# FFT filter and routed experts: ranks, splits and a gather moved in the first expert blocks

## The chip, the cores and the metric

One core of a Trainium2 chip runs the whole program. The metric is the device time of one execution in microseconds (us); lower is better. The kernel before takes 497.0 us in the median of three runs (496.35 to 500.02).

## The reference

```python
X = np.fft.rfft(x, axis=1)                      # x: 8 x 3072 x 256
y = np.fft.irfft(X * (filt_r + 1j*filt_i), n=3072, axis=1)
x = y.reshape(24576, 256)
logits = x @ w_gate                             # 8 experts
idx = argmax(logits); gate_w = softmax(logits)[idx]
# every expert takes the first 768 tokens that chose it (in token order); others give 0
h = relu(disp @ w1)                             # per expert 768x256 @ 256x1024
y = h @ w2                                      # 1024x256
out[i] = gate_w[i] * y[expert of i, slot of i]
```

## The kernel before, in words

The rows of a batch are filtered in stages: a transform of length 128, a transform of length 24 with the product by the filter (`wide`, banks 4 and 5 of PSUM), the inverse, and back to rows. Since each expert takes only 768 tokens, the kernel does three batches (`FIRST = 3`), the third (`t == HALF`, 2) by half, and asks at the end whether all experts are full; the code under `r > 0` is for the case that they are not, and isn't run here.

Behind the batches come 16 expert blocks of 384 tokens (`BLOCKS`, `TOK`), two for each of the 8 experts. `spot(b)` gives expert and half: blocks 0 to 3 are experts 0, 1, 0, 1, then 4 and 5 are expert 2, 6 and 7 expert 3 and so on. Blocks 0 and 1 use only tokens of the first two batches; block 2 is the first that needs the routing of the third. What a block does:

- `pool_gather` (L1143, POOL): three indirect DMAs of 128 rows into `g_in[b % 2]`. It waits until the turn of two blocks before has freed the buffer.
- turn, `pe_block_turn` (L642, TensorE): six transposes into banks 0 and 1; ACT copies them to `xh` (L763), VectorE writes the remainder `xl` (L825).
- up(b) (L1255, TensorE): 8 tiles of 6 matmuls of 384 columns, round four banks (4, 5, 6, 7). The product in fp32 is made of three products of parts (`xh`, `xl` with `w1h`, `w1l`). ACT makes `hh` (L1034) of every tile, VectorE `hl` (L1083). Tile n waits for the `hl` of tile n-4. The turn of block b+1 stands before tile 6 in blocks 0 and 2, and behind up(b) in most others.
- down(b, s) (L1269, TensorE): 24 matmuls for each of three parts s, into banks 2 and 3 in turn; ACT scales by the gates to `o_out` (L1043, `downed`), and POOL stores the rows with an indirect DMA (L1171, `pool_sent`). The gates are fetched by `pool_gates` (L1155).

The weights of an expert are loaded raw by SP (`raw_load`, L981 for w1, L983 for w2; 1 MB each, one raw buffer for w1 and one for w2 from expert 1 on). ACT makes the high part (`act_split`, L995 for w1, L997 for w2), then `low_split` (L1005) the low part: VectorE for w1, POOL for w2 (from expert 1 on). The load for the next expert waits for the low split of the one before, since it overwrites its raw buffer: w1 of expert 3 is loaded only behind the low split of w1 of expert 2. Slot e % 2 of `w1h`, `w1l`, `w2h`, `w2l` holds expert e, so a w1 split of expert 2 may not start before up(2) is done (`h_done`), and a w2 split of expert 2 not before down(2) is done (`o_done`).

Order of the first blocks on TensorE (`pe_last`, `pe_experts`): products 0 to 3 of the third batch (L576, rows of y), turn(0), products 4 and 5, a wait until all y copies are out of banks 0 to 3, the rank matmuls (`pe_rank`, L591 and L592, into bank 3), up(0) with turn(1), up(1), down(0) parts 0 and 1, `pe_table` (L603, makes the token table of the third batch), down(0) part 2, down(1) parts 0 and 1, turn(2), down(1) part 2, up(2) with turn(3), up(3), turn(4), down(2), up(4), turn(5), down(3), and from there up(b), turn(b+1), down(b-1).

VectorE works off the routing of the third batch in `dve_route` steps between the `hl` of blocks 0 and 1 (`FIRST_ROUTE`, `NEXT_ROUTE`): steps 8 and 9 (L873, L877) behind the first `hl`, 10 and 11 behind the second, 12 (L886) and 13 behind the third, up to 21 (L907); the one-hot steps `hot_lo` (L912, three of them), L915, L918, L921 in block 1. `pe_table` waits for the last of them, and the tokens (L946) for gather 2 wait for `pe_table`.

Engine queues are in order. Each order is written by hand, so a wait holds back all that stands behind it in the same queue. POOL's order ahead of block 2: gathers 0 and 1, wait for tile 5 of up(0), gates 0, low split of w2 of expert 1, the store of the third batch's gates, gates 1, stores of block 0, gather 2, gather 3, stores of block 1, wait for tile 6 of up(2), gates 2, wait for tile 2 of up(3), gather 4, wait for tile 7, gates 3.

Of the kernel before, what the change touches and what calls it, by code (L numbers as in the profile page):

```python
# [29 lines left out]
HALF = FIRST - 1  # L30
# [164 lines left out]
def build(nc, x, fab_d, wg, w1, w2, wa_d, wf_d, wbi_d, wai_d, sq_d, tri_d, row_d, num_d, out):  # L195
# [4 lines left out]
    with ExitStack() as ctx:  # L200
# [80 lines left out]
        ps = [psum[:, i].rearrange("p k d -> p (k d)") for i in (0, 1, 4, 5, 2, 3, 6, 7)]  # L281
        work = [psum[:, i].rearrange("p k d -> p (k d)") for i in range(WORK + 1)]
        back = [psum[:, i].rearrange("p k d -> p (k d)")[:, 0:DH * 4 * HR] for i in (3, 6)]
# [160 lines left out]

        held = [None] * (WORK + 1)
        place_of = {"pe": 0, "act": 0}
# [198 lines left out]
        def place_of_row(t, i, engine):  # L645

            return 2 + (i - 4) if t == HALF and i >= 4 else next_work(engine)

        def pe_last(pe, t, r):
            pe_logits(pe, t, 0)  # L650
            pe_logits(pe, t, 1)
            for k, i in enumerate(half_order() if t == HALF else range(N2 // 2)):
                pe_turn_v(pe, t, i)
                if k == 1:
                    pe_raw(pe, t)
                if k == 3:
                    pe_route_in(pe, t)
            for i in range(products(t)):
                if r == 0 and i == 4:
                    for k in range(DH):  # L660
                        free_work(pe, k)
                    pe_block_turn(pe, r, 0)
                pe_product(pe, t, i, place_of_row(t, i, "pe"))
            for k in range(WORK + 1):
                free_work(pe, k)
            if r == 0:
                pe_rank(pe, t, 5)

# [351 lines left out]
        def act_experts(act, r, last):  # L1020
            def turned(b):
                act_block_turned(act, r, b)
# [23 lines left out]
            if r > 0:  # L1046
                turned(0)
            for b in range(BLOCKS):
                q, i = divmod(b, 4)
# [7 lines left out]
                if 0 < b < BLOCKS - 1 and b != 2:  # L1057
                    turned(b + 1)
                if b == 0:
                    act_split(act, r, 1, 1)  # L1060
                if i == 3 and more:
                    act_split(act, r, 2 * q + 3, 0)
                if i == 2 and more:
                    act_split(act, r, 2 * q + 2, 0)
# [4 lines left out]
                if i == 0 and q > 0:  # L1069
                    act_split(act, r, 2 * q + 1, 1)  # L1070
                if i == 3 and more:
                    act_split(act, r, 2 * q + 2, 1)
            downed(BLOCKS - 1)

        def dve_experts(dve, r, last):
# [34 lines left out]
            for b in range(2 if r == 0 else 0, BLOCKS):  # L1110
# [4 lines left out]
                if 0 < b < BLOCKS - 1 and b != 2:  # L1115
                    turned(b + 1)
                if i == 3 and more:
                    low_split(dve, r, 2 * q + 3, 0)
                if i == 2 and more:
                    low_split(dve, r, 2 * q + 2, 0)  # L1120
# [59 lines left out]
        def pool_last(pool, t, r):  # L1180
            gate_store(pool, t - 1)
            if r == 0:
# [5 lines left out]
                pool_gather(pool, r, 1)  # L1188
                pool_after(pool, r, 0, 5)
                pool_gates(pool, r, 0)  # L1190
                low_split(pool, r, 1, 1)
                gate_store(pool, t)
# [11 lines left out]
        def pool_experts(pool, r, last):  # L1204
# [10 lines left out]
            pool_sent(pool, r, 1)  # L1215
            pool_after(pool, r, 2, 6)
            pool_gates(pool, r, 2)
            pool_after(pool, r, 3, 2)
            pool_gather(pool, r, 4)
            pool_after(pool, r, 3, 7)  # L1220
            pool_gates(pool, r, 3)
# [15 lines left out]
        def pe_experts(pe, r, last):  # L1237
# [3 lines left out]
            def up(b):  # L1241
# [4 lines left out]
                for f in range(FT):  # L1246
                    if n * FT + f >= 4:
                        pe.wait_ge(hl_done, n * FT + f - 3)
                    if b in (0, 2) and f == TURN_AFTER:
                        turn(b + 1)  # L1250
# [31 lines left out]
            up(0)  # L1282
            up(1)
            down(0, 0)
            down(0, 1)
# [197 lines left out]
```

## Time and profile before

| what | us |
|---|---|
| median of 3 runs (lowest, highest) | 497.0 (496.35, 500.02) |
| the profiled execution: time | 496.46 |
| the profiled execution: span in the profile | 494.6 |
| TensorE busy | 453.8 (92% of the span) |
| VectorE, ACT, POOL busy | 243.0, 215.4, 188.8 |

The span runs from the first to the last instruction of the profile. Times inside it are counted from its start. "Busy" is the sum of the durations; an engine that is idle while another sets the end costs nothing. The mean granted clock of TensorE is 0.993 of full speed. The chain that ended last is the work followed backwards from the last instruction, at each step to what released it.

### The profile page before, as it was taken

Reading aid. Unit: us, or ns where it says so; the run is one execution under the profiler, and the core shown is the slowest. Engines: PE = TensorE matmul, PEld = TensorE weight load, DVE = VectorE, ACT = ScalarE, POOL = GpSimd, SP = SyncE. Lnnn points to the kernel's source line nnn. Section 1 sums busy time; section 2 is a strip of 40 time slices with the busy share of each in tenths; the row PEclk is TensorE's granted clock in tenths of the full one; section 3 lists DMA queues with packets and bytes.
Section 4 is the critical chain, followed back from the end, with each engine's and each line's share of the span. In section 5 each row is a group of like instructions: output and inputs, shape, how many; then the busy total and the mean of one; then the engine's idle time right before and its main releaser. Section 6 shows DMA issues by size and latency. Waiting matters only on the chain.

```text
span 494.6 us, 12093 instructions
## 1 busy us (share of the span) xinstructions
PE 453.8 (92%) x5160; PEld 399.2 (81%) x5160; DVE 243.0 (49%) x380; ACT 215.4 (44%) x402; POOL 188.8 (38%) x159
## 2 busy tenths in 40 slices
PE   5989999896998878989979999999999999999993
PEld 5855558555774464979969999999999999999993
DVE  1095526899499965791453242363134344224300
ACT  2745555351455546621544253455434345423310
POOL 0000000000000050386467887566786457584122
PEclk9999999998999999999999999999999999999998
DMA  8994989859943354822132794411795310970011
GB/s 301 404 401 137 345 260 323 290 205 329 320 136 120 136 209 129 279 87 86 43 118 66 239 404 167 138 45 33 242 403 184 129 43 27 345 268 23 33 35 36
DMA packets 45743, 93.02 MB, mean 188 GB/s; under 512 B 5840, under 2 KB 20848, under 8 KB 45168
## 3 DMA queue, kind: packets, MB, share of 16 engines
q1 hardware_dynamic: 39408, 79.50, 45.8%
q0 software_dynamic: 6272, 12.65, 7.7%
q8 instruction: 43, 0.70, 0.6%
q14 instruction: 20, 0.16, 0.1%
HBM read 46.49 MB, written 45.64 MB: 186 GB/s over the span
## 4 chain that ended last, share of the span: by engine, by line
PE 79%; DVE 12%; issue 4%; DMA 2%; ACT 1%; POOLq 0%; POOL 0%; SPq 0%; DVEq 0%; ACTq 0%
PE psum L1269 27%; PE psum L1255 25%; DVE prod L787 5%; PE psum L489 4%; PE psum L506 4%; PE psum L473 4%; PE psum L546 3%; PE psum L503 3%; PE psum L642 2%; PE psum L580 2%; PE psum L536 2%; PE psum L522 1%; DVE hot_lo L912 1%; DVE prod L795 1%; PE psum L576 1%
## 5 line engine op out<-in xcount | busy, mean ns | idle before, releaser
L1083 DVE SCALAR_TENSOR_TENSOR hl<-psum,hh 128x384 fp32r<-128x384 f32 x128 | 69.6, 556 | 144.4 <-ACT hh L1034 144.4
L1269 PE MATMUL psum<-w2h,hh 128*128 128x256 f32 x384 | 109.9, 286 | 0.0
L1269 PE MATMUL psum<-w2h,hl 128*128 128x256 f32 x384 | 108.8, 283 | 0.0
L1269 PE MATMUL psum<-w2l,hh 128*128 128x256 f32 x384 | 108.8, 283 | 0.0
L1034 ACT ACTIVATE hh<-psum 128x384 fp32r<-128x384 f32 x128 | 62.1, 492 | 61.5 <-PE psum L1255 61.3
L1255 PE MATMUL psum<-xh,w1h 128*128 128x384 f32 x256 | 86.2, 337 | 2.1 <-DVE hl L1083 2.0
L1255 PE MATMUL psum<-xh,w1l 128*128 128x384 f32 x256 | 85.7, 335 | 0.0
L1255 PE MATMUL psum<-xl,w1h 128*128 128x384 f32 x256 | 85.7, 335 | 0.0
L787 DVE TENSOR_TENSOR prod<-psum,fab 128x1024 f32<-128x1024 f32 x48 | 56.5, 1218 | 47.2 <-PE psum L473 38.9
L1171 POOL DMA_INDIRECT out<-o_out,token x48 | 50.2, 1047 | 70.5 <-ACT o_out L1043 56.7
L1269 PEld LDWEIGHTS psum<-w2l,hh 128*128 128x128 f32 x384 | 73.7, 192 | 0.0
L1269 PEld LDWEIGHTS psum<-w2h,hh 128*128 128x128 f32 x384 | 73.6, 192 | 0.0
L1269 PEld LDWEIGHTS psum<-w2h,hl 128*128 128x128 f32 x384 | 73.6, 192 | 0.0
L1143 POOL DMA_INDIRECT g_in<-y_rows,token x48 | 53.5, 1115 | 46.6 <-DVE token L946 32.3
L1043 ACT ACTIVATE o_out<-psum,o_gate 128x256 f32<-128x256 f32 x48 | 22.8, 475 | 108.3 <-PE psum L1269 108.3
L1155 POOL DMA_INDIRECT o_gate<-gate_rows,token x48 | 50.1, 1044 | 35.4 <-PE psum L1255 21.8
L1134 POOL DMA_DIRECT2D gate_rows<-gate x2 | 1.3, 660 | 145.3 <-DVE carry L883 145.3
L1255 PEld LDWEIGHTS psum<-xh,w1h 128*128 128x128 f32 x256 | 48.1, 188 | 3.0 <-DVE hl L1083 2.6
L1255 PEld LDWEIGHTS psum<-xl,w1h 128*128 128x128 f32 x256 | 48.1, 188 | 0.0
L1255 PEld LDWEIGHTS psum<-xh,w1l 128*128 128x128 f32 x256 | 48.1, 188 | 0.0
L489 PEld LDWEIGHTS psum<-wbi,prod 64*64 64x64 f32 x1536 | 34.4, 136 | 16.7 <-issue 9.8
L489 PE MATMUL psum<-wbi,prod 64*64 64x96 f32 x1536 | 39.5, 251 | 7.2 <-issue 3.3
(109 smaller groups left out, 540.7 us busy)
## 6 DMA issues: line engine op xcount, KB each, us to landing
out<-zero SPq DMA_DIRECT2D x24, 1024.0 KB, 12.3
w_raw<-in_w SPq DMA_DIRECT2D x14, 1024.0 KB, 5.8
x_in<-in_x SPq DMA_DIRECT2D x18, 512.0 KB, 6.4
t_scratch<-t_out SPq DMA_DIRECT2D x24, 256.0 KB, 4.1
z_in<-t_scratch SPq DMA_DIRECT2D x32, 192.0 KB, 3.9
y_rows<-y SPq DMA_DIRECT2D x12, 512.0 KB, 2.8
fab<-in_fab SPq DMA_DIRECT2D x4, 1024.0 KB, 14.4
first_raw<-in_w SPq DMA_DIRECT2D x2, 1024.0 KB, 8.2
```

Source lines behind the costliest of these rows:

```text
L473: mm = nc.tensor.matmul(wide[q * QR:(q + 1) * QR, a, c, :], wf[part(a), NQ * h + q, c, :], z_in[part(a), n % ZB, q, :], start=True, stop=True)
L489: mm = nc.tensor.matmul(back[q][part(low), at:at + 2 * HR], prod[part(q), n % 2, 0, a, c, d:d + A1], wbi[part(q), j, a, c, :], start=(c == ...
L506: mm = nc.tensor.matmul(work[k][:, :], wa[:, :], x_in[:, c, 2 * h:2 * h + 2, :], start=True, stop=True)
L787: nc.vector.tensor_tensor(prod[:, n % 2, f], wide, fab[:, h, :, f, :].unsqueeze(2).to_broadcast([P, 2, 2, D]), ALU.mult).then_inc(p_done, 1)
L1034: nc.scalar.activation(hh[:, b % 2, f, :], ps[(2, 3, 6, 7)[f % 4]][:, 0:TOK], ACT.Relu).then_inc(hh_done, 1)
L1043: nc.scalar.activation(o_out[:, b % 2, s, :], ps[4 + (b * ST + s) % 2][:, 0:D], ACT.Copy, scale=o_gate[:, b % 4, s:s + 1]).then_inc(o_evac, 1)
L1083: nc.vector.scalar_tensor_tensor(out=hl[:, b % 2, f, :], in0=ps[(2, 3, 6, 7)[f % 4]][:, 0:TOK], scalar=0.0, in1=hh[:, b % 2, f, :].bitcast ...
L1143: nc.gpsimd.indirect_dma_start(out=g_in[:, b % 2, s, :], out_offset=None, in_=yd[0:have], in_offset=bass.IndirectOffsetOnAxis(ap=tokens_of ...
L1155: nc.gpsimd.indirect_dma_start(out=o_gate[:, b % 4, s:s + 1], out_offset=None, in_=gd[0:have], in_offset=bass.IndirectOffsetOnAxis(ap=toke ...
L1171: nc.gpsimd.indirect_dma_start(out=out, out_offset=bass.IndirectOffsetOnAxis(ap=tokens_of(r, b, s), axis=0), in_=o_out[:, b % 2, s, :], in ...
L1255: mm = nc.tensor.matmul(ps[(2, 3, 6, 7)[f % 4]][:, 0:TOK], wt[k][:, h, f * P:(f + 1) * P], xx[:, b % 2, h, :], start=(m == 0), stop=(m == 5))
L1269: mm = nc.tensor.matmul(ps[4 + (b * ST + s) % 2][:, 0:D], hx[:, b % 2, f, s * P:(s + 1) * P], wt[k][:, f, :], start=(f == 0 and m == 0), s ...
```

## The change

- Banks: products 4 and 5 of the third batch go to banks 4 and 5 in place of 2 and 3. The rank matmuls go right behind turn(0), ahead of products 4 and 5, still in bank 3, which no product uses any more. The wait for all y copies ahead of them is gone; up(0) waits before tile 0 for the copy out of bank 4 and before tile 1 for that out of bank 5, and down(0) waits for banks 2 to 5.
- The w2 split of expert 1 (ACT) goes from behind the `hh` of block 0 to ahead of them. The low split that follows it on POOL goes ahead of gates 0, and POOL's wait for tile 5 of up(0) is gone.
- Gather 4 goes from behind tile 2 of up(3) to right behind the stores of block 1, ahead of gates 2; the waits for tile 6 of up(2) and tile 7 of up(3) are gone, that for tile 2 of up(3) stands now ahead of gates 3.
- The w1 split of expert 2 (ACT, and the low split on VectorE) goes from behind up(2) to behind up(3) and its turn(4). The w1 split of expert 3 goes on ACT from ahead of the `o_out` of block 2 to behind them, ahead of the w2 split of expert 2; its low split on VectorE goes from behind the `hl` of block 3 to behind those of block 4 and the `xl` of turn(5).

```diff
--- before.py
+++ after.py
@@ -279,7 +279,7 @@
 
         psum = ctx.enter_context(nc.psum_tensor("psum", [P, 8, 2, D], F32))
         ps = [psum[:, i].rearrange("p k d -> p (k d)") for i in (0, 1, 4, 5, 2, 3, 6, 7)]
-        work = [psum[:, i].rearrange("p k d -> p (k d)") for i in range(WORK + 1)]
+        work = [psum[:, i].rearrange("p k d -> p (k d)") for i in range(6)]
         back = [psum[:, i].rearrange("p k d -> p (k d)")[:, 0:DH * 4 * HR] for i in (3, 6)]
         wide = psum[:, 4:6]
         raw_at = P
@@ -442,7 +442,7 @@
                 for n in range(NG - 1, FIRST_ZEROS):
                     zeros(sp, n)
 
-        held = [None] * (WORK + 1)
+        held = [None] * 6
         place_of = {"pe": 0, "act": 0}
 
         def next_work(engine):
@@ -644,7 +644,7 @@
 
         def place_of_row(t, i, engine):
 
-            return 2 + (i - 4) if t == HALF and i >= 4 else next_work(engine)
+            return i if t == HALF and i >= 4 else next_work(engine)
 
         def pe_last(pe, t, r):
             pe_logits(pe, t, 0)
@@ -660,11 +660,11 @@
                     for k in range(DH):
                         free_work(pe, k)
                     pe_block_turn(pe, r, 0)
+                    pe_rank(pe, t, 5)
                 pe_product(pe, t, i, place_of_row(t, i, "pe"))
-            for k in range(WORK + 1):
-                free_work(pe, k)
-            if r == 0:
-                pe_rank(pe, t, 5)
+            if r > 0:
+                for k in range(WORK):
+                    free_work(pe, k)
 
         def act_a(act, t, i, first):
             c, h = divmod(i, 2)
@@ -1045,6 +1045,7 @@
 
             if r > 0:
                 turned(0)
+            act_split(act, r, 1, 1)
             for b in range(BLOCKS):
                 q, i = divmod(b, 4)
                 more = q < E // 2 - 1
@@ -1056,11 +1057,9 @@
                     downed(1, range(2))
                 if 0 < b < BLOCKS - 1 and b != 2:
                     turned(b + 1)
-                if b == 0:
-                    act_split(act, r, 1, 1)
-                if i == 3 and more:
+                if i == 3 and q > 0 and more:
                     act_split(act, r, 2 * q + 3, 0)
-                if i == 2 and more:
+                if i == 2 and q > 0 and more or b == 3:
                     act_split(act, r, 2 * q + 2, 0)
                 if b == 1:
                     downed(1, range(2, ST))
@@ -1068,6 +1067,8 @@
                     downed(b - 1)
                 if i == 0 and q > 0:
                     act_split(act, r, 2 * q + 1, 1)
+                if b == 3:
+                    act_split(act, r, 3, 0)
                 if i == 3 and more:
                     act_split(act, r, 2 * q + 2, 1)
             downed(BLOCKS - 1)
@@ -1114,9 +1115,9 @@
                     upped(b, f)
                 if 0 < b < BLOCKS - 1 and b != 2:
                     turned(b + 1)
-                if i == 3 and more:
-                    low_split(dve, r, 2 * q + 3, 0)
-                if i == 2 and more:
+                if i == 3 and q > 0 and more or b == 4:
+                    low_split(dve, r, 3 if b == 4 else 2 * q + 3, 0)
+                if i == 2 and q > 0 and more or b == 3:
                     low_split(dve, r, 2 * q + 2, 0)
 
         def tokens_of(r, b, s):
@@ -1186,9 +1187,8 @@
                 rows_ready(pool, t)
                 pool_gather(pool, r, 0)
                 pool_gather(pool, r, 1)
-                pool_after(pool, r, 0, 5)
+                low_split(pool, r, 1, 1)
                 pool_gates(pool, r, 0)
-                low_split(pool, r, 1, 1)
                 gate_store(pool, t)
                 pool_gates(pool, r, 1)
             else:
@@ -1213,11 +1213,9 @@
             pool_sent(pool, r, 0, range(ST - 1, ST))
             pool_gather(pool, r, 3)
             pool_sent(pool, r, 1)
-            pool_after(pool, r, 2, 6)
+            pool_gather(pool, r, 4)
             pool_gates(pool, r, 2)
             pool_after(pool, r, 3, 2)
-            pool_gather(pool, r, 4)
-            pool_after(pool, r, 3, 7)
             pool_gates(pool, r, 3)
             for b in range(2, BLOCKS - 1):
                 q, i = divmod(b, 4)
@@ -1246,6 +1244,8 @@
                 for f in range(FT):
                     if n * FT + f >= 4:
                         pe.wait_ge(hl_done, n * FT + f - 3)
+                    elif n == 0 and f < 2:
+                        free_work(pe, 4 + f)
                     if b in (0, 2) and f == TURN_AFTER:
                         turn(b + 1)
                     if b == 2 and f == 3:
@@ -1281,6 +1281,9 @@
                 turn(0)
             up(0)
             up(1)
+            if r == 0:
+                for k in range(2, 6):
+                    free_work(pe, k)
             down(0, 0)
             down(0, 1)
             if r == 0:
```

## Rows read from the trace of the kernel before

**Rows 1.** Chain that ended last, in order of time: start us, us, what
```profile
192.31 0.84 PE psum L642 x6
...
195.07 0.59 ACT y L723
...
196.75 6.38 PE psum L1255 x36
...
210.49 3.49 DVE hot_lo L912
213.98 1.40 DVE hl L1083 x3
...
218.61 1.37 DVE hot_eq L915
...
222.90 1.18 PE psum L603 x24
...
252.59 4.95 DMA g_in<-y_rows,token
...
258.46 8.63 PE psum L1269 x72
267.10 8.33 PE psum L1255 x48
```

**Rows 2.** Windows: length, busy us by engine (count), granted TensorE clock, DMA share, GB/s
```profile
255.00:260.00 5.00, 2.48 (x22) 2.42 (x22) 1.73 (x4) 2.32 (x4) 3.78 (x5) 1.00 0.11 33
300.00:494.00 194.00, 186.42 (x1346) 185.93 (x1344) 61.43 (x102) 75.82 (x141) 108.96 (x93) 0.99 0.39 136
```

**Rows 3.** Waits of TensorE, 185 to 300 us: us in total, times, longest
```profile
PE psum L642 <- DMA g_in<-y_rows,token: 2.5, 1, 2.5
PE psum L1255 <- DVE hl L1083: 2.0, 2, 1.0
PE psum L603 <- DVE hot_hi L921: 1.3, 1, 1.3
PE psum L591 <- ACT y L723: 1.1, 1, 1.1
```

**Rows 4.** ACT in order of time: start us, us, line, what [idle before <-releaser]
```profile
197.96 0.49 ACT L1034 ACTIVATE hh<-psum 128x384 fp32r<-128x384 f32 x1 [2.31 <-PE psum L1255]
...
206.30 1.91 ACT L997 CAST w2h<-w_raw 128x2048 fp32r<-128x2048 f32 x1
...
267.19 0.48 ACT L1043 ACTIVATE o_out<-psum,o_gate 128x256 f32<-128x256 f32 x1 [2.40 <-PE psum L1269]
...
269.36 1.39 ACT L1034 ACTIVATE hh<-psum 128x384 fp32r<-128x384 f32 x3
```

**Rows 5.** POOL in order of time, same columns
```profile
208.29 4.61 POOL L1005 TENSOR_TENSOR w2l<-w_raw,w2h 128x2048 fp32r<-128x2048 f32 x1 [1.85 <-ACT w2h L997]
...
243.50 1.03 POOL L1155 DMA_INDIRECT o_gate<-gate_rows,token  x1 [4.55 <-PE psum L1255]
...
252.59 1.00 POOL L1143 DMA_INDIRECT g_in<-y_rows,token  x1 [0.30 <-issue]
```

**Rows 6.** VectorE, lines L912 and L903: duration ns min/median/max, first and last start us
```profile
L912 DVE TENSOR_TENSOR hot_lo<-small,nums x9: 1211/1224/3572, 102.3 to 217.4; 128x1024 bf16<-128x1024 f32 x9
...
L903 DVE TENSOR_SCALAR small<-small x3: 178/178/321, 101.7 to 204.8; 128x24 f32<-128x24 f32 x3
```

**Rows 7.** VectorE in order of time, columns as in rows 4
```profile
198.96 0.17 DVE L873 TENSOR_SCALAR small<-small 128x24 f32<-128x24 f32 x1
...
201.05 0.35 DVE L886 TENSOR_TENSOR lg<-lg,base 128x192 f32<-128x192 f32 x1
...
204.90 1.02 DVE L825 TENSOR_TENSOR xl<-psum,xh 128x384 fp32r<-128x384 f32 x2
```

**Rows 8.** Landing of L981's loads: the one at 250.2 us, then at 199.6 us
```profile
DMA to landing us min/median/max: 4.9/4.9/4.9
...
DMA to landing us min/median/max: 9.4/9.4/9.4
```

## The prediction

> **What bounds the kernel now.** I read first the chain of work that ended last, in order of time [rows 1]. From 192 us on it is mostly TensorE: up blocks of 8.33 us (48 matmuls of L1255), down blocks of 8.63 us (72 of L1269), a turn between. The reader is to see the places where another engine stands in it: ACT's last y copy, VectorE's `hl` and then `hot_lo` for 3.49 us, a gather of 4.95 us. The windows [rows 2] say why only these count: from 300 us TensorE is busy 186.42 of 194 us, and the chain there is TensorE alone, so up(4), which starts at 267.10, fixes the end. The forecast is by how much that start moves. The waits of TensorE [rows 3] price what is to be had: 2.5 us for a gather, 2.0 us in two waits for `hl`, 1.3 us for the one-hot table, 1.1 us for `y`.
>
> **Ranks and banks.** Today the rank matmuls wait for the copy that starts at 195.07 [rows 1] and up(0) is under way at 196.75. With products 4 and 5 in banks 4 and 5 and the ranks in bank 3 right behind the turn, TensorE waits for nothing there: turn at 192.31 for 0.84, products done by 195.07, where the copy of the last starts, and the ranks between them, which take 0.6 today (the copy ends at 195.65, 0.5 to the restart, up(0) at 196.75), so up(0) starts at 195.7. That is 0.9 us, the 1.1 us wait less a restart. VectorE's `xl` is done at 195.5, so no more is to be had. The two new bank waits of up(0) are met: the copies of products 4 and 5 come about 0.5 us later than now (ranks ahead of them), to about 195.4 and 196.2, and banks 4 and 5 are first written at 195.7 and 196.7. The waits for banks 2 to 5 ahead of down(0) are met 16 us before. Behind up(0) waits nothing else.
>
> **The w2 split of expert 1 on ACT.** It moves from 206.30 to behind the last y copy: 196.1 to 198.0, at its 1.91 us [rows 4]. So the first `hh` comes at 198.0, where it is now (197.96), although TensorE was 0.9 us ahead: the gain of the ranks is swallowed here, and VectorE starts its chain of `hl` and route steps at 198.5 as before. That chain has next to no gaps until `xl` at 204.90 to 205.92 [rows 7], which releases up(1) at 206.0.
>
> **The low split of w2 on POOL.** It takes 4.61 us [rows 5], now 208.29 to 212.90; it waits for the ACT split, so it goes to 198.1 to 202.7. What is late next: `hl` 1 ends at 203.8 in place of 200.1, so TensorE stands about 2.9 us before the sixth tile of up(0); `xl` ends at 209.4 and up(1) starts there, 3.4 us late. `hl` of its third tile, 210.49 at its end now, ends at 213.9; the first `hot_lo` at its undisturbed 1.14 ends at 215.0; then five `hl` 0.47 apart, two `hot_lo` and three steps of 1.37, 1.38 each with the gap [rows 1], 8.8 us, and about 0.55 in waits for `hh`: the last ends at 224.35, against 222.77 now. The pe_table at 222.90 [rows 1] starts **1.6 us later**, and gather 2 and turn(2) hang on it through the tokens, all late by the same. If L873 passes and only L886 waits, up(1) starts at 207.65 and the table comes 0.2 us earlier. If neither waits it comes 2.0 us earlier.
>
> The Trainium skill (SBUF — State Buffer, Who interferes with whom) says that the pair of ports that VectorE shares with GpSimd is held for a whole instruction, that a two-input VectorE instruction contends with a GpSimd one that reads SBUF, and that copies and tensor_scalar can contend too. The `hot_lo` row agrees with the first two; by the third L873 waits, which is the value taken; without it the sum is 1.8 us lower.
>
> Gates 0 behind the low split are issued from 202.9 to 206.7 and wanted by the first `o_out`, behind all of up(1): hidden, with some 10 us to spare before they would hold ACT; gates 1 likewise.
>
> **The first w1 split behind up(3).** Gone from between up(2) and up(3): ACT 1.9 and VectorE 2.29, which made `hl` late and cost TensorE the second 1.0 us wait [rows 3], 1.17 us from tile to tile.
>
> **The fifth gather.** Gather 4 now waits for tile 2 of up(3) and for gates 2; its last part is issued at 252.59 [rows 5] and turn(4) starts at 257.59. Moved behind the stores of block 1, which end at 238.95 (POOL is idle for the 4.55 us from there to gates 2), its three parts go at 239.3 to 242.9, 1.0 and a gap of 0.3 each [rows 5]; turn(2), which frees the buffer, lies before that. With the landing that it has now it is there by 247, 6 us ahead of turn(4). TensorE gets back the 2.5 us, 2.6 with the restart, and a turn of 0.66 in place of 0.87. Gates 2 and 3 behind it end at 251, wanted at 261: hidden. Together with the split: turn(4) at 257.59-2.6-1.17 = 253.8 by the present times, down(2) at 254.5 where it now starts at 258.46, so **4.0 us less**.
>
> **The two w1 splits that arrive behind up(3).** Let T be the start of turn(4). ACT: last `hh`, `xh`, then split of w1 2 to T+3.4; VectorE's low split (2.29) to T+5.75. Only then is the raw buffer free, and SP issues the load of w1 3, 1 MB: 4.9 us alone, 9.4 us beside the zero stores [rows 8]. Nothing else of size runs, so I take 4.9: it lands at T+10.7. ACT's last `o_out` of down(2) ends at T+9.9 (0.57 behind TensorE, as 267.19+0.48 to 267.10 now [rows 1, 4]) and the next in its queue is the split of w1 3. It waits to T+10.7, ends at T+12.6, the w2 split behind it at T+14.45, the first `hh` of up(4) behind both, its `hl` at T+15.4 (0.95 us behind the split: 0.49 and 0.56, less the overlap of a tenth that `hh` has with the split before it). TensorE wants that `hl` before the fifth tile of up(4), at T+0.66+8.63+4.17 = T+13.46. So a new stall of **2.0 us** stands where today is a margin of about 0.9 (first `hl` at 270.4, fifth tile at 271.27). With the load at no cost it is 1.1; with 9.4 us it is 6.5. POOL's low split of w2 2 slips by about 3 us and with it gates 4, 5 and gather 6: those go to T+31.4, while turn(6) is at T+37.5; 6 us for a landing of 3 to 5 are enough. VectorE's low split of w1 3 lies in the 9 us of down(3).
>
> **The sum**: +1.6 -4.0 +2.0 = -0.4 us. The profiled execution has a span of 494.6 and a time of 496.46, 1.9 us around it; the median of the runs is 497.0, half a microsecond above. From the profiled one: **496.1 us**.
>
> **The rivals.**
> A (forecast, 0.52): L873 waits for POOL; -0.4, 496.1. For it: the two slowed rows. Against: L903 lost only 0.14 us beside a POOL instruction of 0.99.
> B (0.25): small single-input steps pass, L886 waits 1.7 us: -0.2 -4.0 +2.0 = -2.2, 494.3. For it: the blocked row is of L886's kind. Against: L903.
> C (0.10): none of the small steps waits, only long ones do, so POOL's new place is free: -2.0 -4.0 +2.0 = -4.0, 492.5. Against: the wait of `hot_lo` came at its start, whatever its length.
> D (0.10), slower: the load of w1 3 is late. Its path has no slack: each microsecond over 4.9 goes into the stall of up(4). From 5.3 us on it outweighs the gain of A; at 9.4 us the time is 496.1 + 4.5 = 500.6. For it: the load of w1 2 took 9.4. Against: the zero stores that slowed it come later here.
> E (0.03): gather 4 lands no earlier, because POOL is late through its other work: -0.4 +2.6 = +2.2, 498.7. Against: POOL is idle 4.55 us ahead of gates 2.
> A long stall could also lower TensorE's clock; a stretch with 2.48 of 5 us busy kept 1.00 [rows 2], so I give it nothing.
>
> **Range and chances.** A, B and C span 492.5 to 496.1; a load of 5.8 or a gather that slips add one to two, and the runs differ by some 0.3 below C, so 492.2 to 499.0 holds near 0.85. A measurement of this kernel tells about 1%, 5 us, from no change: only C with a microsecond more is faster than that (0.07), only D at its worst slower (0.04), 0.89 lie between.
>
> **What would show it.** Right: up(0) at 195.7; POOL's low split at 198 to 202.7 and L873 of nearly 4 us; `hot_lo` at 1.2 everywhere; the table near 224.5; no wait at turn(4), none for `hl` in up(3); a wait of 2 us for `hl` in up(4) behind ACT's w1 3 split. Wrong: L873 at 0.17 and L886 long (B), both short (C), the split of w1 3 waiting far behind its load (D), a gather still in the chain (E).

## The result and the profile after

The changed kernel is a little slower. Beside each other on one chip, 20 executions each, the median is 500.56 us (495.96 to 503.52) against 496.96 for the kernel before, 3.6 us more. The ratio of the two kernels, taken without the executions that lie clearly above the rest and not from the medians, is 1.0053, 95% interval 1.003 to 1.0075, so +2.6 us. The profiled execution took 500.54 us, its span is 498.7. In a later comparison the same kernel came out at 1.0009 (0.997 to 1.0048), which is no change (e6 below), so the loss is small and its size not the same everywhere. The forecast was 496.1, range 492.2 to 499.0.

The span is 4.1 us longer, but turn(0) already starts at 195.92 us, 3.6 later than the 192.31 of [rows 1], and nothing ahead of it was changed. TensorE's granted clock has two low stretches there that the first trace of the kernel before has not (0.66 in 40 to 45 us and in 95 to 100). So I count from turn(0): 302.29 us to the end of the span before, 302.78 after. A second trace of each (e5, e6 below) has 300.8 and 303.6.

The chain of work that ended last, after, in order of time (start us, us, what), beside [rows 1]:

```profile
195.92 0.85 PE psum L642 x6
...
199.62 1.80 ACT w2h L997
...
202.31 3.81 DVE small L873
...
206.92 1.54 PE psum L1255 x6
...
227.68 1.18 PE psum L603 x24
...
259.04 8.64 PE psum L1269 x72
...
290.12 7.28 DMA g_in<-y_rows,token
...
297.44 0.87 PE psum L642 x6
```

Counted from turn(0) the table (L603) comes at 31.76 in place of 30.59 (1.2 later; I had 1.6), down(2) at 63.1 in place of 66.15 (3.0 earlier; I had 2.4), turn(6) at 101.5 in place of 100.6. What is new in the chain is first ACT's w2 split, which stands ahead of the first `hh`, then L873, and last a gather that takes 7.28 us from the start of its POOL instruction to its landing.

The waits of TensorE after, from 185 to 310 us (total, times, longest), beside [rows 3]:

```profile
PE psum L1255 <- DVE hl L1084: 4.1, 2, 2.2
PE psum L642 <- DMA g_in<-y_rows,token: 1.6, 1, 1.6
PE psum L603 <- DVE hot_hi L921: 0.8, 1, 0.8
```

The 1.1 us for `y` is gone, and the 2.5 us at turn(4). The two waits for `hl` are others than before, 2.2 in up(0) and 1.9 in up(4), and the gather waited for is gather 6, not 4.

VectorE, POOL and ACT in order of time (start us, us, line, what, and in brackets the idle time before it and what ended it), beside [rows 4, 5, 7]:

```profile
202.31 3.80 DVE L873 TENSOR_SCALAR small<-small 128x24 f32<-128x24 f32 x1
```

```profile
201.50 4.58 POOL L1005 TENSOR_TENSOR w2l<-w_raw,w2h 128x2048 fp32r<-128x2048 f32 x1 [11.10 <-ACT w2h L997]
...
280.20 3.11 POOL L1156 DMA_INDIRECT o_gate<-gate_rows,token  x1 [0.30 <-issue]
```

```profile
268.99 1.91 ACT L995 CAST w1h<-w_raw 128x2048 fp32r<-128x2048 f32 x1 [0.74 <-DMA w_raw<-in_w]
270.80 1.90 ACT L997 CAST w2h<-w_raw 128x2048 fp32r<-128x2048 f32 x1
272.61 1.62 ACT L1034 ACTIVATE hh<-psum 128x384 fp32r<-128x384 f32 x4
```

L873, 0.17 us before, takes 3.80, and ends 0.03 us behind POOL's low split (201.50+4.58 = 206.08). On POOL also the last part of gates 4 takes 3.11 us in place of 1.0; it begins with VectorE's low split of the w1 of expert 3 (280.15 to 282.43). The kernel before has the same between other instructions, a part of gather 5 that takes 2.72 us beside the low split of the w1 of expert 3:

```profile
261.30 2.72 POOL L1143 DMA_INDIRECT g_in<-y_rows,token  x1 [0.30 <-issue]
```

```profile
260.86 2.29 DVE L1005 TENSOR_TENSOR w1l<-w_raw,w1h 128x2048 fp32r<-128x2048 f32 x1 [1.15 <-ACT w1h L995]
```

On ACT, in the changed kernel, the w1 split of expert 3 starts 0.74 us late, waiting for its load, the w2 split stands right behind it, and `hh` of up(4) only then.

L912 after (duration ns min/median/max), beside [rows 6]: no instance waits any more.

```profile
L912 DVE TENSOR_TENSOR hot_lo<-small,nums x9: 1216/1220/1226, 106.5 to 222.1; 128x1024 bf16<-128x1024 f32 x9
```

TensorE's clock behind turn(0): windows of 5 us (length, busy of PE, PEld, DVE, ACT, POOL, granted clock, DMA share, GB/s).

```profile
205.00:210.00 5.00, 3.08 (x14) 2.98 (x15) 4.86 (x13) 1.44 (x4) 4.24 (x4) 0.78 1.03 340
210.00:215.00 5.00, 5.00 (x26) 4.75 (x25) 4.12 (x12) 1.83 (x5) 4.08 (x6) 0.87 1.04 354
```

The clock falls, between its levels of 2.4 and 1.2 GHz, behind the wait of 2.21 us in up(0).

### The profile page after: what moved, and what is told of

It is laid out like the page before. It is cut to its first block, busy times and chain, and to the rows that moved or that the text cites. A ratio compares the mean times of both kernels' runs of the same rounds, so it can differ in the third digit from the quotient of the medians.

```text
span 498.7 us, 12091 instructions
## 1 busy us (share of the span) xinstructions
PE 458.2 (92%) x5160; PEld 401.8 (81%) x5160; DVE 244.4 (49%) x380; ACT 215.8 (43%) x402; POOL 186.4 (37%) x159
## 4 chain that ended last, share of the span: by engine, by line
PE 75%; DVE 12%; issue 6%; DMA 2%; POOL 2%; ACT 1%; POOLq 0%; SPq 0%; DVEq 0%; ACTq 0%
PE psum L1269 25%; PE psum L1255 22%; DVE prod L787 5%; PE psum L506 5%; PE psum L489 4%; PE psum L473 3%; PE psum L546 3%; PE psum L503 3%; PE psum L580 3%; PE psum L642 2%; PE psum L536 2%; DMA g_in<-y_rows,token 1%; PE psum L522 1%; POOL o_gate L1156 1%; DVE prod L795 1%
## 5 line engine op out<-in xcount | busy, mean ns | idle before, releaser
L1144 POOL DMA_INDIRECT g_in<-y_rows,token x48 | 50.3, 1047 | 45.1 <-DVE token L946 31.8
L1156 POOL DMA_INDIRECT o_gate<-gate_rows,token x48 | 51.1, 1064 | 15.3 <-issue 13.9
```

The costliest lines, as they stand in the source:

```text
L1144: nc.gpsimd.indirect_dma_start(out=g_in[:, b % 2, s, :], out_offset=None, in_=yd[0:have], in_offset=bass.IndirectOffsetOnAxis(ap=tokens_of ...
L1156: nc.gpsimd.indirect_dma_start(out=o_gate[:, b % 4, s:s + 1], out_offset=None, in_=gd[0:have], in_offset=bass.IndirectOffsetOnAxis(ap=toke ...
```

## The experiments

Theories. **1**: POOL's low split of w2 in its new place holds VectorE up at L873, which makes a hole in up(0), and the lower clock behind it costs more. **2**: the w1 split of expert 3 on ACT holds back `hh` of up(4), and through POOL gather 6. **3**, formed behind e7: gather 6 lands late beside the zero stores. The first four runs share a chip, so do the next four and the last four. On the first of these chips the kernel before takes 516.57 us in the median, and the traces of e1, e2 and e3 have waits that those of the other chips lack, the first in up(2) (2.90, 1.40 and 1.79 us). So I use those four traces up to turn(2), and of e3 also up(4) and up(5). The changed kernel was not run there, so what e1 to e4 expected of its time, and of the ends of the traces, stays open. All times "from turn(0)" are read from the traces.

**e1_undo_w2.** The splits of w2 of expert 1 back in their old places.

```diff
-            act_split(act, r, 1, 1)          # ahead of block 0
+                if b == 0:                    # behind upped(0)
+                    act_split(act, r, 1, 1)
...
-                low_split(pool, r, 1, 1)
+                pool_after(pool, r, 0, 5)
                 pool_gates(pool, r, 0)
+                low_split(pool, r, 1, 1)
```

> The changed kernel, with the w2 split of expert 1 on ACT, its low split on POOL and POOL's wait for tile 5 put back where they were before. I count from the start of turn(0), since what lies ahead of it is not touched: to the table 30.6 us in the kernel before and 31.8 in the changed one, to the end of the span 302.3 and 302.8. Theory 1 (the hole that L873 leaves in up(0), with TensorE's clock lower behind it, costs the block): L873 back at 0.17 us, hot_lo again up to 3.5, clock 1.00 from 195 to 220 us, table at 29.7 (0.9 earlier than before the change, the ranks' gain), end at 300.8, time 1 to 3 us under the changed kernel. Rival (the loss is all at up(4) and turn(6)): table moves by under 0.5, end stays at 302.8, time as the changed kernel.

Measured: table at 29.58 (expected 29.7), no wait in up(0), L912 again up to 3557 ns:

```profile
L912 DVE TENSOR_TENSOR hot_lo<-small,nums x9: 1207/1224/3557, 102.8 to 218.5; 128x1024 bf16<-128x1024 f32 x9
```

Ratio to the kernel before 1.0043 (0.9994 to 1.0092), median 518.04, so no gain in the total shows. The cost at the table is settled: against its old place, the new place of the split costs 31.76 - 29.58 = 2.2 us there.

**e2_reduce_873.** L873 another kind of instruction.

```diff
-                ins = nc.vector.tensor_scalar(norm, total, 1e-9, None, ALU.add)
+                ins = nc.vector.tensor_reduce(norm, total.unsqueeze(2), AX.X, ALU.add)
```

> The changed kernel, with L873 alone made another kind of instruction: a reduce over one element in place of the tensor_scalar (it leaves out the addition of 1e-9 to a sum of at least 1). Theory 1 (a single-input tensor_scalar uses the ports that POOL's split holds, a reduce does not): L873 short; then the next of a blocked kind waits. If that is the reciprocal L877: 3.4 us there, nothing gained. If it is L886, two inputs: about 1.7 us, table 30.4 us behind turn(0) instead of 31.8, clock near 1.00 in up(1), time 1 to 3 us under the changed kernel. Rival (anything of VectorE that starts beside POOL's split from SBUF waits, whatever its kind): the reduce takes 3.8 us, all else as in the changed kernel.

Measured, VectorE and POOL in order of time:

```profile
201.15 0.17 DVE L873 TENSOR_REDUCE small<-small 128x24 f32<-128x24 f32 x1
201.35 0.30 DVE L877 RECIPROCAL gate<-small 128x24 f32<-128x24 f32 x1
...
202.72 2.45 DVE L886 TENSOR_TENSOR lg<-lg,base 128x192 f32<-128x192 f32 x1
```

```profile
200.34 4.61 POOL L1005 TENSOR_TENSOR w2l<-w_raw,w2h 128x2048 fp32r<-128x2048 f32 x1 [13.02 <-ACT w2h L997]
```

The reduce takes 0.17 us in the middle of POOL's split, the reciprocal its usual 0.30, two sums with one input in PSUM pass, and L886, the first with two inputs in SBUF, waits for POOL's end at 204.95: 2.45 in place of 0.35. Table at 30.34 (expected 30.4). So of two instructions of the same shape in the same place the kind decides: the tensor_scalar waited, the reduce does not. The rival falls. TensorE's hole moves from up(0) to the start of up(1), 2.61 us there. Ratio 0.9997 (0.9962 to 1.0031), median 515.07.

By the Trainium skill (SBUF — State Buffer, Who interferes with whom) copy, cast and tensor_scalar can contend with GpSimd, a tensor_reduce never does on trn2, and a tensor_tensor does with both inputs in SBUF; the rows of this case agree in all three (3.80 us for L873, 0.17 for the reduce, 2.45 for L886).

**e3_w13_late**, and on the next chip **e7_w13_late**. The w1 split of expert 3 behind the `o_out` of block 3.

```diff
-                if b == 3:
+                if b == 4:
                     act_split(act, r, 3, 0)
```

> The changed kernel, with the w1 split of expert 3 on ACT moved from ahead of the w2 split of expert 2 to behind the o_out of block 3. Theory 2 (that split waits for its load and holds back ACT's queue; through it the stall in up(4), and through POOL's late low split the wait for gather 6 at turn(6)): no wait for hl in up(4) (2.2 now), no wait at turn(6) (1.6 now), from up(4) to the end 227.5 us as before the change in place of 231.0, time 3 to 3.5 us under the changed kernel. Rival (turn(6) waits because the zero stores run later against gather 6, not because of POOL's queue): the 2.2 goes and the 1.6 stays, time 2 under.

> The changed kernel with the w1 split of expert 3 behind the o_out of block 3, once more beside the kernel before and the changed one. Theory 2: no wait for hl in up(4), turn(5) 17.6 us behind turn(4) (19.8 in the changed kernel), no wait at turn(6), time 2 to 3.5 us under the changed kernel. Rival: the split now holds ACT in block 5 instead, so a wait for hl of 1 to 2 us in up(5), and the time is that of the changed kernel.

Measured: the wait in up(4) is gone, turn(5) stands 17.6 us behind turn(4) in both (19.8 to 20.0 in the changed kernel). In both the loss comes back one block later, as e7's rival said: in e7 2.85 us in up(5), turn(6) at 102.3 and no wait there, in e3, on the chip with the other waits, 5.80 us in up(5). Ratio 1.0004 (0.9964 to 1.0043), median 514.91 for e3; 1.005 (1.0014 to 1.0086), median 501.31 for e7, where the changed kernel has 498.23 (e6). No gain. ACT, VectorE, TensorE's wait and the landing of gather 6 in e7:

```profile
286.01 1.90 ACT L997 CAST w2h<-w_raw 128x2048 fp32r<-128x2048 f32 x1
287.81 1.90 ACT L995 CAST w1h<-w_raw 128x2048 fp32r<-128x2048 f32 x1
289.61 1.62 ACT L1034 ACTIVATE hh<-psum 128x384 fp32r<-128x384 f32 x4
```

```profile
289.74 2.29 DVE L1005 TENSOR_TENSOR w1l<-w_raw,w1h 128x2048 fp32r<-128x2048 f32 x1 [11.44 <-ACT w1h L995]
291.95 1.94 DVE L1084 SCALAR_TENSOR_TENSOR hl<-psum,hh 128x384 fp32r<-128x384 f32 x4
```

```profile
PE psum L1255 <- DVE hl L1084: 5.1, 2, 2.8
```

```profile
DMA to landing us min/median/max: 2.8/2.8/2.8
```

Two splits, 3.6 us together, stand between ACT's last `o_out` and its first `hh`. VectorE adds to that: the edit left its low split of the w1 of expert 3 where it was, ahead of the `hl` of block 5, so VectorE stands still for 11.44 us and then does the low split before the first `hl`, which starts at 291.95, though its `hh` begins at 289.61. In the changed kernel, where no low split is in between, the first `hl` of up(4) starts 0.5 us behind the start of its `hh`. By that, an estimate, about 1.8 of the 2.85 us are VectorE's order and 1.0 is ACT's. e3 also has a use for the clock. It has the same hole in up(0) (2.23 us) and no lower clock behind it (windows as above):

```profile
205.00:210.00 5.00, 3.45 (x23) 3.13 (x22) 4.86 (x14) 2.23 (x5) 4.39 (x5) 1.00 1.00 323
```

and the table comes at 31.76, to the hundredth as in the first trace with 0.78 and 0.87. TensorE, at the full clock, has a wait of 1.55 us at the start of up(1) instead. The lower clock costs nothing there, since VectorE sets the pace of block 1; that half of theory 1 falls.

**e4_both_free.** As e3, and the low split of w2 of expert 1 on VectorE behind the tokens, ACT's split behind block 0 (of the edit only the low split is shown).

```diff
-                low_split(pool, r, 1, 1)      # POOL; now nc.vector for expert 1
...
                 both()
+                low_split(dve, r, 1, 1)
                 turned(2)
```

> The changed kernel with both suspected costs taken out: the w1 split of expert 3 behind the o_out of block 3, and the w2 split of expert 1 on ACT behind block 0 as before, its low split on VectorE behind the tokens in place of POOL ahead of them. Theories 1 and 2 together: no POOL split beside the route steps, so hot_lo 1.2 and L873 0.17; table about 28.3 us behind turn(0) (30.6 before, 31.8 changed), low split of w2 done about 26 us before down(1) stalls or up to 0.5 us late, no waits in up(4) and at turn(6), clock 1.00 from turn(0) on; end about 296 us behind turn(0), 6 us (1.2%) under the kernel before. Rival (VectorE was not the bound of blocks 0 and 1, TensorE's own work is): table at 29.7, end at 297.5.

Measured: table at 27.87 (expected 28.3), 3.9 us earlier than in the changed kernel and 1.7 earlier than in e1: so much does POOL's split cost at the table in its new place and in its old one. But 1.1 us come back as a wait of down(1) for the low part and 2.2 at turn(2), at 41.3 where the changed kernel has 41.5. Beside VectorE's split the first part of gather 2 takes 2.24 us instead of 1.0, POOL's row first, then VectorE's:

```profile
229.77 2.24 POOL L1146 DMA_INDIRECT g_in<-y_rows,token  x1 [2.26 <-DVE token L946]
```

```profile
228.81 2.29 DVE L1005 TENSOR_TENSOR w2l<-w_raw,w2h 128x2048 fp32r<-128x2048 f32 x1
```

and the load of w2 of expert 2, which waits for this split, now runs beside the gather. That these two make the wait at turn(2) is my reading: the trace names nothing that ended it. Ratio 0.9945 (0.9908 to 0.9982), median 512.6, so 2.8 us under the kernel before; the traced execution is a longer one, 517.29 us.

**e5_before** and **e6_after**: both kernels unchanged.

> The kernel before, unchanged, for a second trace of it, with its clock by execution. Theory 1 (the hole that L873 leaves in up(0) brings a lower clock into block 1): clock 1.00 from turn(0) to turn(4), and any lower stretches lie in the batch stages ahead of turn(0). Rival (lower stretches fall anywhere by chance): one of them within 30 us of turn(0). The share of executions with a mean clock under 0.985 tells which: few by theory 1, most by the rival.

> The changed kernel, unchanged. Theory 1: again a stretch of lower clock (0.7 to 0.9 in a 5 us window) 10 to 20 us behind turn(0), table at 31.8, and most executions at a mean clock 0.010 under those of the kernel before. Theory 2: wait for hl of 1.9 in up(4), gather 6 late at turn(6) by 0 to 2. Rival: the lower stretch in block 1 of the first trace was chance; then the clock is 1.00 there and the table comes at 31.0 or less, since about 0.7 us of the 31.8 would be the clock.

Measured: e5 498.67 us, 1.0001 (0.9965 to 1.0037), end 300.8 from turn(0); e6 498.23 us, 1.0009 (0.997 to 1.0048), table 31.78, end 303.6, clock 0.76 and 0.89 in the windows behind the hole. The same clock in both by execution: a mean of 0.9860 over 12 for the kernel before and 0.9856 for the changed one, four of each under 0.985. So on this chip the change does not lower the mean clock, against what theory 1 expected. The waits of e6 (total, times, longest) and the landing of gather 6:

```profile
PE psum L1255 <- DVE hl L1084: 4.4, 2, 2.2
PE psum L642 <- DMA g_in<-y_rows,token: 2.1, 2, 1.8
```

```profile
DMA to landing us min/median/max: 5.6/6.1/7.5
```

**e8_gathers_only.** e1's and e7's edits together.

> The changed kernel with both parts that I hold for costs undone or put off: the w2 split of expert 1 and its low split on POOL in their old places, the w1 split of expert 3 behind the o_out of block 3. What stays is the ranks, gather 4 and the w1 split of expert 2 behind up(3). Theories 1 and 2: table 29.6 behind turn(0), turn(4) at 60.2, no waits from there, end 297.3 behind turn(0), 5 us (1.0%) under the kernel before. Rival (the gain of gather 4 is lost later, to transfers that come closer together): end at 300 or more.

Measured: table 29.6, turn(4) 60.3, turn(5) 77.9, all as expected, and then turn(6) at 100.1, where the kernel before has it (100.1 in e5), since 2.85 us of waiting in up(5) as in e7 come first. Ratio 0.9992 (0.9951 to 1.0033), median 497.9. The 4.6 us won by turn(5) are all lost in one block. TensorE there, and the window of its clock:

```profile
286.29 0.69 PE L1257 MATMUL psum<-xh,w1h 128*128 128x384 f32 x1 [2.85 <-DVE hl L1085]
...
287.09 0.52 PE L1257 MATMUL psum<-xh,w1l 128*128 128x384 f32 x1
287.41 0.52 PE L1257 MATMUL psum<-xh,w1h 128*128 128x384 f32 x1
...
290.27 0.33 PE L1257 MATMUL psum<-xh,w1l 128*128 128x384 f32 x1
290.45 0.33 PE L1257 MATMUL psum<-xh,w1h 128*128 128x384 f32 x1
```

```profile
285.00:290.00 5.00, 3.71 (x13) 3.72 (x14) 3.18 (x6) 0.49 (x1) 4.37 (x4) 0.66 0.61 141
```

Here the lower clock has a price. Behind the wait the matmuls start 0.32 us apart, from 289.6 on 0.17 apart. The ten from 286.29 on take 3.29 us in place of about 1.7, so about 1.6 of the 4.6 us are the clock (an estimate from these rows), which nothing hides where TensorE itself sets the pace.

**f1_zeros_late.** The zero stores of a pair of experts behind the w2 load.

```diff
+                if q < E // 2 - 1:
+                    raw_load(sp, r, 2 * q + 2, 1)
                 if q > 0 and r == 0:
                     for k in range(PER_PAIR):
...
                 if q < E // 2 - 1:
-                    raw_load(sp, r, 2 * q + 2, 1)
```

> The changed kernel, with the five zero stores of 1 MB that SP issues behind the w1 load of expert 4 put behind the w2 load of expert 4 (the same for the later pairs). Theory 3 (gather 6 is issued as I worked out, but lands 6 to 7 us later in place of 3, because it runs beside the zero stores; so the 1.65 and 1.85 us wait at turn(6)): gather 6 lands in 3 us, no wait at turn(6), turn(6) 100.5 behind turn(0) where the changed kernel has 101.5 and 102.5, the wait of 2 us in up(4) stays. Rival (POOL is late with gather 6): wait at turn(6) stays at 1.6 or more.

Measured: no wait at turn(6), which comes at 99.9, though gather 6 is issued at the same distance behind turn(4) within half a microsecond; instead 0.9 us at turn(7), beside which the stores now run. Ratio 1.0009 (0.9976 to 1.0042), median 498.63.

```profile
PE psum L1256 <- DVE hl L1085: 4.1, 2, 2.2
PE psum L642 <- DMA g_in<-y_rows,token: 0.9, 1, 0.9
```

So the stores make gather 6 late. Theory 3 holds for the wait. Moving the stores moves the wait on to gather 7, and the end comes at 302.7, as in the first trace of the changed kernel.

**f2_w13_block4.** The w1 split of expert 3 in ACT's idle time of block 4.

```diff
                 if i == 2 and q > 0 and more or b == 3:
                     act_split(act, r, 2 * q + 2, 0)
+                if b == 4:
+                    act_split(act, r, 3, 0)
...
-                if b == 3:
-                    act_split(act, r, 3, 0)
```

> The changed kernel, with the w1 split of expert 3 on ACT in block 4 behind the xh of turn(5) and ahead of the o_out of block 3, where ACT is idle for 2.4 us; in e7 it stood behind them, back to back with the w2 split, and held hh for 3.7 us. Theory 2 (a split costs TensorE nothing alone in a block, 2 to 4 us when two stand together ahead of hh): no wait for hl in up(4) nor in up(5), turns 17.6 apart from turn(4) on, turn(6) at 97.6 behind turn(0) if gather 6 is in time; its wait there may be 0 to 2. Time 2 to 4 us under the changed kernel. Rival (a second w1 split anywhere in blocks 3 to 5 costs the same): a wait of 2 us in up(5).

Measured: turns 17.6 apart from turn(4) at 62.4 on, turn(6) at 97.6, end 298.8 (302.8 and 303.6 in the changed kernel). Ratio 0.9971 (0.9938 to 1.0004), median 496.15, so the gain is seen in the trace and not quite clear in the total. ACT, all waits of TensorE of over 0.8 us, and the landing of gather 6:

```profile
274.76 1.93 ACT L995 CAST w1h<-w_raw 128x2048 fp32r<-128x2048 f32 x1
277.25 0.47 ACT L1043 ACTIVATE o_out<-psum,o_gate 128x256 f32<-128x256 f32 x1 [0.56 <-PE psum L1269]
...
283.36 1.90 ACT L997 CAST w2h<-w_raw 128x2048 fp32r<-128x2048 f32 x1
```

```profile
PE psum L1255 <- DVE hl L1084: 2.2, 1, 2.2
PE psum L603 <- DVE hot_hi L921: 0.8, 1, 0.8
```

```profile
DMA to landing us min/median/max: 5.5/6.0/6.6
```

The split lies between `xh` and the first `o_out`, which is not delayed. The zero stores still run beside gather 6 here, and it still lands slowly, but its last part starts 28.3 us behind turn(4) in place of 31.7, so it is there in time.

**f3_best.** f2 and e1 together.

> As f2_w13_block4, and with the w2 split of expert 1 and its low split in the places of the kernel before. Theories 1 and 2: table 29.6, turn(4) 60.3, turn(5) 77.9, turn(6) 95.5 behind turn(0) or up to 2 later through gather 6, end at 297.3 to 299; 3.5 to 5 us (0.7 to 1.0%) under the kernel before. Rival (gains ahead of turn(6) are lost there, because the zero stores and gather 6 don't move with TensorE): turn(6) at 100, end as before the change.

Measured: table 29.57, turn(5) 78.1, turn(6) 95.7, end 296.7. Ratio **0.9894** (0.9859 to 0.9929), median 492.52 of 8 executions: 5 us under the kernel before, the lowest ratio of all. The traced execution is the longest of the 8 (497.22 us); its turn(0) comes late, at 198.72, and what is gained shows behind it. Its waits of TensorE behind turn(0), those of over 0.8 us:

```profile
PE psum L603 <- DVE hot_hi L921: 1.3, 1, 1.3
PE psum L1257 <- DVE hl L1085: 1.0, 1, 1.0
```

**f4_gather_only.** Gather 4 alone in the kernel before.

```diff
-            pool_after(pool, r, 2, 6)
+            pool_gather(pool, r, 4)
             pool_gates(pool, r, 2)
             pool_after(pool, r, 3, 2)
-            pool_gather(pool, r, 4)
-            pool_after(pool, r, 3, 7)
```

> The kernel before with gather 4 alone moved (behind the stores of block 1, gates 2 behind it, wait for tile 2 of up(3) ahead of gates 3). The splits stay where they were. By my sum this is worth 2.8 us: no wait at turn(4), down(2) 2.6 us earlier and a shorter turn, the 1.0 us wait in up(3) and all else as before: turn(4) 62.6, turn(5) 80.2, turn(6) 97.8 behind turn(0), time 2.5 to 3 us under the kernel before. Rival (turn(6) waits for its gather beside the zero stores): turn(6) at 99 or more.

Measured: turn(4) 62.7, turn(5) 80.3, turn(6) 97.9, end 298.7, no wait at turn(4), the other waits as before. Ratio 0.9974 (0.994 to 1.0009), median 495.64, which does not rule out no change. In the trace it is worth 2.7 us at turn(6), close to the 2.8 summed.

## Why the prediction was wrong

The number was 496.1 and no change clear of the noise; measured is 500.56, and +0.5% by the ratio. By its steps:

- **Ranks and banks: right.** up(0) starts 3.3 us behind turn(0), 4.3 before, and the gain is swallowed by ACT's split: the first `hl` comes 5.9 behind turn(0), 6.2 before.
- **POOL's low split, case A: right.** L873 3.80 us (I had 3.7), `hot_lo` 2.35 us back, the table 1.2 later (I had 1.6). It was a choice between two bounds, with a chance of 0.52: no row had a tensor_scalar beside a POOL instruction of that length. e2 shows the mechanism, and cases B and C fall. B's price for the table (0.2 earlier than before) fits what e2 made of it: 30.34 against 30.59. The hole in up(0) is 2.2 us, I had 2.9.
- **First w1 split and gather 4: right.** No wait in up(3) nor at turn(4); from the table to down(2) 31.4 us in place of 35.6, 4.2 less (I had 4.0). f4 prices the gather alone at 2.6 to 2.7.
- **The stall of up(4): right.** 1.89 us and 2.14 (I had 2.0), with the load landing in 5.0 us and ACT waiting 0.74 for it. D did not come.
- **The failed step is the sentence on gather 6.** "6 us for a landing of 3 to 5 are enough." From the start of its last part to its landing it took 7.28 us (in e6 the three parts land in 5.6 to 7.5, 6.1 in the median), since the zero stores run beside it. In e7, where the stores go out behind it, it lands in 2.8; in f2, where they run beside it, in 5.5 to 6.6. I took the landing from the quiet gathers, though the stores run beside gather 6 in the kernel before too: the five of this pair start from 275.5 us on and land in 11.0 to 17.2. The prediction's T+31.4 does not say whether it is the start or the end of the last part's instruction; measured, it starts 31.7 us behind turn(4) (290.12 - 258.38) and ends at 32.7. In the kernel before it starts at 27.2. Of the 4.5 us between, 2.5 are POOL's low split, which waits for ACT's late w2 split (I had 3), and 2.1 the gates fetch stretched to 3.11 us beside VectorE's low split, which I had not seen, though the trace of before has the 2.72 us shown above. Late issue and slow landing both have to be there: f1 takes away the stores, f2 most of the delay, and in both the wait is gone. turn(6) was due at T+37.5, the gather is there at T+39.0. The term is +1.65 us in the first trace, +1.85 in e6, none in f1. With it the sum of -0.4 becomes +1.3 to +1.5; at turn(6) the traces have +1.0 in the first pair and +2.3 in e5 and e6.
- **The share ahead of turn(0)** is not explained by the change, and without it the number would have lain in the range: with the failed step put right the sum gives 497.7 to 497.9. In the first pair of traces 3.6 of the 4.1 us lie ahead of turn(0). In the first comparison 15 of 20 executions of the changed kernel have a mean clock under 0.985, beside e5 4 of 12 (e6), as many as of the kernel before. In the first comparison the five executions with a higher clock take 495.96 to 498.12 us, the fifteen others 499.34 to 503.52; for the kernel before only one clock of that comparison is on record, 0.993. What makes low stretches of the clock frequent in the batch stages of one kernel's executions on one chip was not found, and I can't say how much of the 2.6 us it is. The traces behind turn(0) give between +0.5 and +2.8 us.
- **The range** ended at 499.0 because D, the only way there was to 500, needed a late load. The transfer that was late was another one, which I had set down as hidden.

Where did the gain go? 4.2 us are won between the table and down(2), less 1.2 lost to L873. Then ACT, which has now two splits ahead of the `hh` of up(4), takes 2 of them, and gather 6 takes 1.7 more. The last two come from the order in the queues, not from the work: f2 has the same instructions and is 4.0 us shorter in the trace.

## What to carry to other kernels

Cost a moved instruction by what it lands beside: look at the queue of the engine that it can hold up, at its new time, kind by kind, and at every transfer issued within its slip. In this kernel ACT's queue, with an `hh` every microsecond, bears one 1.9 us split in a block, best where it waits anyway, and not two back to back. Move the partner of a split along with it: VectorE's low split, left behind in e7, held VectorE's whole queue. When a bound is moved forward by some microseconds, list every transfer that does not move with it and take its landing from rows of the same traffic.

## What the runs showed of the hardware

- Beside a POOL tensor_tensor of 4.6 us, VectorE instructions differ by kind. A tensor_scalar of 24 elements waited to its end (3.80 us in place of 0.17), so did a tensor_tensor with both inputs in SBUF (2.45 in place of 0.35); a tensor_reduce (0.17), a reciprocal (0.30) and instructions with one input in PSUM did not wait. That the reciprocal is free I had not expected.
- The other way round POOL gives way too: an indirect DMA's instruction took 2.24 us (e4) and 3.11 us (the changed kernel) in place of 1.0 beside VectorE's low split of 2.29 us, and 2.72 in the kernel before.
- An indirect gather of 128 rows landed in 2.8 us alone (e7) and in 5.5 to 7.5 us beside the 1 MB zero stores (f2, e6).
- TensorE's granted clock fell behind a wait of 2.2 us in up(0) in five of the six traces that have one (0.66 to 0.78), not behind the 2.5 us at turn(4) of the kernel before; in f4 and e5 it was 1.00 from turn(0) to turn(4). The table came at the same time with it and without (31.75 to 31.78), since VectorE set the pace. Behind the 2.85 us in up(5) of e8, where TensorE sets the pace, the lower clock cost about 1.6 us (estimate above).
